# Constant matmuls into a spare PSUM bank, placed where the tensor engine waits in the convolution stage

## What is computed

```python
out = np.einsum('hk,bskhg->bshg', softmax(weight), x_unfolded)   # convolution
logits = x @ w_gate;  e = argmax(logits);  gate_w = softmax(logits)[e]
out = gate_w * (relu(x @ w1[e]) @ w2[e])                         # layer 1
out = gate_w * sigmoid((x @ w_output_gate)[e]) * (relu(x @ w1[e]) @ w2[e])  # layer 2
```

## Time and profile before

| | |
|---|---|
| median of 3 runs | 1430.34 us (1422.12 to 1433.67) |
| the profiled execution | 1426.65 us |
| its span, first to last instruction | 1425.1 us |
| PE busy over the span | 1248.3 us (88%) |
| DVE, ACT, POOL busy | 860.8 (60%), 641.3 (45%), 445.0 us (31%) |
| mean granted TensorE clock | 0.913 |

### The profile page before, as it was taken

One profiled execution on the slowest core, in us unless ns is written; L12 is line 12 of the kernel. 1 busy time (PEld: TensorE's weight loads), 2 busy tenths in 40 slices (PEclk: granted clock), 3 DMA queues, 4 the chain that ended last, 5 costly groups with the idle time before them and its releaser, 6 DMA issues.

```text
span 1425.1 us, 38152 instructions
## 1 busy us (share of the span) xinstructions
PE 1248.3 (88%) x13162; PEld 1169.3 (82%) x13162; DVE 860.8 (60%) x2298; ACT 641.3 (45%) x1126; POOL 445.0 (31%) x476
## 2 busy tenths in 40 slices
PE   2876763299989999999999991999999999999998
PEld 2765663298979998999999990899999999999997
DVE  3787885358978998887777774333333333333332
ACT  3666664045545555554444441333333333333332
POOL 1366777412323333322222222122222222222222
PEclk9666655599999999999999995999999999999999
DMA  8388674928585858561515113462425525125510
GB/s 232 103 254 265 199 224 145 261 65 218 149 235 141 251 146 240 144 203 42 146 40 148 40 35 94 115 156 44 137 63 142 128 64 152 44 44 151 152 44 16
DMA packets 204695, 194.94 MB, mean 137 GB/s; under 512 B 147359, under 2 KB 179771, under 8 KB 199522
## 3 DMA queue, kind: packets, MB, share of 16 engines
q1 hardware_dynamic: 176352, 127.72, 34.8%
q0 software_dynamic: 26096, 64.50, 14.5%
q10 hardware_dynamic: 2194, 2.06, 0.5%
HBM read 101.38 MB, written 70.80 MB: 121 GB/s over the span
## 4 chain that ended last, share of the span: by engine, by line
PE 72%; DVE 12%; DMA 6%; issue 4%; another core or an unknown queue 2%; ACT 2%; POOL 2%; SPq 1%; POOLq 0%; DVEq 0%; ACTq 0%
PE bank L720 70%; DMA wslot<-image 3%; DVE am L943 2%; PE bank L725 2%; POOL rows L466 2%; DVE split L1027 1%; DVE wslot L1054 1%; DVE wam L1012 1%; DVE split L1030 1%; DMA image<-split 1%; DMA stage<-in_moe_w 1%; DVE rowab L952 1%; ACT conv L564 0%; ACT rowt L564 0%
## 5 line engine op out<-in xcount | busy, mean ns | idle before, releaser
L720 PE MATMUL bank<-xT,wslot 128*128 128x256 f16 x5040 | 639.5, 275 | 59.2 <-DMA xT<-rows 50.1
L1114 DVE SCALAR_TENSOR_TENSOR hl<-bank,hh 128x512 f16<-128x512 f32 x504 | 347.7, 690 | 417.6 <-ACT hh L653 372.6
L720 PEld LDWEIGHTS bank<-xT,wslot 128*128 128x128 f16 x5040 | 485.5, 99 | 110.0 <-DMA xT<-rows 50.2
L653 ACT ACTIVATE hh<-bank 128x512 f16<-128x512 f32 x504 | 300.6, 596 | 535.9 <-PE bank L720 529.6
L720 PE MATMUL bank<-wslot,hh 128*128 128x192 f16 x4032 | 541.0, 246 | 0.4 <-DVE hl L1114 0.4
L720 PE MATMUL bank<-wslot,hl 128*128 128x192 f16 x2016 | 496.7, 246 | 0.0
L720 PEld LDWEIGHTS bank<-wslot,hh 128*128 128x128 f16 x4032 | 369.8, 98 | 11.8 <-issue 0.8
L552 POOL DMA_INDIRECT out_tokens<-y,idxt x126 | 122.5, 972 | 416.6 <-ACT y L664 348.6
L487 POOL DMA_INDIRECT rows<-rowt,idxp x126 | 130.1, 1032 | 358.0 <-PE bank L720 197.7
L720 PEld LDWEIGHTS bank<-wslot,hl 128*128 128x128 f16 x2016 | 197.6, 98 | 0.1
L466 POOL DMA_INDIRECT rows<-rowab,idxa x96 | 109.3, 1138 | 61.7 <-issue 46.1
(11 more groups left out here) (137 smaller groups left out, 873.9 us busy)
## 6 DMA issues: line engine op xcount, KB each, us to landing
wslot<-image SPq DMA_DIRECT2D x32, 1024.0 KB
wslot<-image SPq DMA_DIRECT2D x32, 768.0 KB
image<-split POOLq DMA_DIRECT2D x18, 512.0 KB
image<-split SPq DMA_DIRECT2D x8, 1024.0 KB
image<-split POOLq DMA_DIRECT2D x9, 768.0 KB
xw<-in_x SPq DMA_DIRECT2D x4, 1536.0 KB
stage<-in_moe_w SPq DMA_DIRECT2D x8, 768.0 KB
image<-split SPq DMA_DIRECT2D x8, 768.0 KB
```

What stands on the lines that cost most here:

```text
L653: nc.scalar.activation(hh[:, c, :], bank[c][:, :], ACT.Relu).then_inc(hh_out, 1)
L720: return nc.tensor.matmul(o, a, b_, start=start, stop=stop, skip_group_check=True)
L1114: V.scalar_tensor_tensor(hl[:, c, :], bank[c][:, :], 0.0, hh[:, c, :], ALU.max, ALU.subtract).then_inc(hl_out, 1)
```

## The change

A function `fill(count)` is added to PE's program. It runs `count` matmuls with `ident` as the stationary and `tri`, repeated four times, as the moving operand, 128 by 512 float16, into bank 4. Nobody reads bank 4, and the fills neither wait for nor raise a semaphore. They are called at three kinds of places: 12 behind round r = 0 and the ranks, 8 behind round r = 1, and one in each of the eight rounds of transposes and logits, behind the logits. With both, every full step has 28 more matmuls (12 + 8 + 8). The wait for `consts` moves from the first logits to the head of PE's program.

```diff
+FILLS = (12, 8)
...
-        RB, YB = 5, 6
+        FILL, RB, YB = 4, 5, 6
...
+            def fill(count):
+
+                for _ in range(count):
+                    mm(bank[FILL][:, :].rearrange("p (r c) -> p r c", r=4), ident[:, :],
+                       tri[:, :].unsqueeze(1).broadcast_to((P, 4, P)), True, True)
+
+            pe.wait_ge(consts, 2)
             pe.wait_ge(band_loaded, 16)
...
                     if r == 0 and late(n, 2):
                         step_ranks(n - 2)
+                    fill(FILLS[r])
                 if late(n, 1):
                     step_logits(n - 1)
...
                 if not late(n, 1):
                     pe.wait_ge(gate_ready, 1)
-                    pe.wait_ge(consts, 2)
...
                     if r:
                         round_logits(r - 1)
+                    fill(1)
                 round_logits(RTR - 1).then_inc(logit_done, 1)
```

## The result

The changed kernel took 1440.07 us, the median of 20 runs (1431.96 to 1451.42); the kernel before, run beside it, 1432.76 us (20 runs, 1422.0 to 1445.92). The ratio is 1.0069, with a 95% interval of 1.0045 to 1.0092: by the medians 7.3 us slower, by the ratio 10 (6 to 13). The profiled execution took 1440.66 us, its span is 1439.0 us and its mean granted clock 0.940.

The account below looks back on a forecast made before the run. A step was taken as DVE's work plus a 4.2 us wait tied to the scatter, not PE. Terms 0 + 0 + 2.4 + 0.9 = +3.3 us gave 1430.0 or 1433.6, 1432 taken; own range 1424 to 1440, full range 1404 to 1441.

Parts of the forecast that it names:

- Price of a fill: One 128x512 float16 matmul on PE: 0.22 us at full clock, 0.40 us at half.
- The start: First steps, where PE is on the chain: fills delay r = 1 and step 1's transposes; +2.4 us taken.
- 12 fills in a steady step: Behind r = 0 and the ranks: 107.0 to 109.6 us at full clock, hidden before the next round at 112.74; 0.
- The lag does not hang on PE: The 4.2 us between ranks' end and `posm` was read as tied to the running scatter, 25 us behind its start.
- the first rival: The lag hangs on PE and fills remove it: up to 23.3 us faster, 1408 or 1413 us; chance 0.22.
- The idle time before r = 1: Sign that the forecast is right: PE's 5.74 us of idle before that convolution round shrinks to about 3.
- The end. [...] I take 0.9: Last eight rounds of logits: fills delay `idxa` to 245.7 or 247.1, POOL's last scatter starts at 245.64; 0.1 to 1.5 us.
- the upper of the two bounds: Eight fills at the stage's end put logits and ranks 1.8 to 3.2 us later; 3.2 is at half clock.
- One fill per round, eight per step. [...] 0: Steady transposes and logits: at half clock logits end 3.2 us later, DVE 1.0 us late at most, covered by its wait; 0.
- 8 fills behind r = 1: Steady step: fills end at 119.4, transposes 0.7 us late, covered by 0.78 us of slack; 0, at worst 0.7 us.
- From 92.9 to 106.6 us: PE's clock stays at half although PE is busy 13.35 of 13.7 us with transposes and small logits.
- The clock's own gain: Full clock saves up to 2.6 us a round, some 34 us of PE over 13 slow rounds; counted as 0.

Follow-up runs that it names:

- hidden_12: The changed kernel with only the 12 fills behind round r = 0 from step 2 on, against the kernel before: 1414.08 us, ratio 0.9977.
- hidden_12_twice: The 12 fills behind round r = 0 of steps 2 to 7 alone, run once more, against the kernel before: 1416.26 us, ratio 1.0001.
- after_again: The changed kernel, unchanged, run again on a chip with late PE signals, against the kernel before: 1442.2 us, ratio 1.009.
- steady_only: The changed kernel with 168 of 224 fills, only in the steady steps and none at the two ends, against the kernel before: 1418.11 us, ratio 1.0012.
- after_third: The changed kernel with all 224 fills, on a chip without late signals of ranks or logits, against the kernel before: 1419.86 us, ratio 1.0036.
- before_again: The kernel before, unchanged, run again for its trace on a chip with late PE signals: 1434.65 us, ratio 1.0018.
- The separate halves: Against the kernel before: the 168 fills of the steady steps alone, 1418.11 us, 1.0012; the other 56, at the two ends, alone, 1419.13 us, 1.0032.
- load_first: The kernel before with SP issuing the next expert weights' load ahead of the store of the split ones, no fills: 1434.77 us, ratio 1.0021.
- bridge_20: Fills in the steady steps only, with 20 instead of 8 behind round r = 1, against the kernel before: 1416.31 us, ratio 0.9997.
- warm_end_40: 12 fills behind round r = 0 of steps 2 to 7 plus 40 before the last transposes, against the kernel before: 1418.21 us, ratio 0.9998.

## Why the prediction was wrong

The range of 1404 to 1441 us held the 1440.07, by 0.9 us, and the change is within 1% as most of the chance had it. But the forecast was +3.3 us with an own range to 1440, and the measured change is 6 to 13 us. By its steps:

- **Price of a fill: right.** Forecast 0.22 and 0.40 us; measured 0.216 at full clock and, from rounds of 1.48 us with a fill and 1.07 without, 0.41 at half.
- **The start: right.** Forecast +2.4 us and `am` of step 1 at 48.5; it started at 48.49, and the fills there put the first read of ranks 2.35 us later over all traces (1.7 in the profiled pair).
- **12 fills in a steady step: 0, right.** hidden_12 and hidden_12_twice measure 0.9977 and 1.0001. Their level was read wrong: they were to take 2.6 us at full clock, and in after two groups of twelve took 3.68 and 3.93 us. A faster round r = 0 leaves PE standing before the ranks, 2.62 us in that step, and the clock is at half behind it (106.9 to 110.3 us).
- **The lag does not hang on PE: right**, and it bore the forecast: the first rival, with its 0.22, did not happen. In after_again the wait before `posm` occurs six times with 4 us and more, with rounds r = 0 at full clock and fills behind the ranks, and the distance from the scatter's first DMA stays at 25 us through all the experiments. The idle time before r = 1 shrank from 5.74 us to 0.47 rather than 3, partly because the twelve fills took 3.93 us in that step.
- **"The end. [...] I take 0.9": the first step that failed**, a term of the sum mis-sized. It measured 2.5 us over all traces and 4.2 in the profiled pair. Two readings went into it. The clock: PE stands 12 us before the last transposes, and the window from 216 us on in the trace of before would have shown 0.50, so that the upper of the two bounds, 3.2 us, was the one to take. The cover: `idxa` was followed to 247.1 us and set against POOL's start at 245.64, but POOL's first DMA starts 0.9 us behind `idxa` (254.06 to 254.96 in the trace of after), and the trace of before had the same:

```profile
112.27 0.17 DVE L1003 CAST idxa<-pos 112x16 int32<-112x16 f32 x1
113.33 0.96 POOL L466 DMA_INDIRECT rows<-wslot,idxa  x1 [3.95 <-DVE idxa L1003]
```

247.1 + 0.9 - 245.64 is 2.4 us, close to what the end costs. That it is so close is partly luck: the fills made the last logits 2.5 us longer (12.22 against 9.70), not 3.2, and the 0.8 us of cover that POOL's queue gave was there in the trace of before alone; in the other eight traces without fills at the end the last scatter starts 2.1 us behind the eighth read, as soon as `idxa` lets it. The further 1.6 us of the pair are the late signal, which the later logits ran into.

- **"One fill per round, eight per step. [...] 0": failed in one step of six** of the profiled execution, at 3.7 us, and in none of after_again. The sum had DVE "1.0 us late at most", with the wait of 4.2 us behind it. It rested on logits that are read promptly, as they were in the trace of before; that a later logits' signal can fall into the late stretch itself was not asked, although that stretch had been read as tied to the scatter and not to the ranks. The prediction's own 104.0 us for logits at half clock is 18.0 us behind the scatter's first DMA at 86.04, well inside it.
- **8 fills behind r = 1: 0, right in its sum** as far as is known. steady_only, which has them beside others, measures 1.0012, and in the long step the transposes waited for DVE and not for the fills. Its side effect was missed: a faster round before a start that is fixed elsewhere makes the stand longer, and the clock fell behind it.
- **A row was read too simply.** From 92.9 to 106.6 us PE was said to be busy "with transposes and small logits"; from 100.63 on it was the round r = 0. That a light load doesn't bring the clock back rests on the part up to there.
- **The clock's own gain: 0, right.** The Trainium skill ("TensorE: Matmul & The Clock Gate", section "Why this matters for your kernels") advises keeping TensorE busy so that its clock stays up. The clock did go up, from 0.65 to 0.82 in the stage, and the kernel lost: the advice is about PE's speed, and PE's speed isn't what the steady part of the stage waits for. The size of the gain in PE's own time was set too high: 34 us, where 16 rounds of 2.85 us leave 75.4 - 45.6, some 30, to be had, and 23 came.

With 2.4 for the end the sum would have been +4.8 us, which is what the prompt chips show (after_third: 1.0036, 5.1 us). **What stays open** is the rest on the slow-signal chips, where the ratios are 1.0069 and 1.009. In after_again against before_again the stage explains 5.8 us, and no place for more was found, in an execution that was the fastest of its kernel; the expert layers differ between executions by more than the few us in question. The intervals of the two kinds of chip overlap (1.0012 to 1.006 against 1.0045 to 1.0092), so that a larger loss with slow signals is likely, by the long step above, but not shown. The separate halves were measured on prompt chips only.

## What to carry to other kernels

Fill an engine's standing time only where its next start is set elsewhere and late enough, and leave out every place where it is on the chain, above all the first and the last pass of a pipeline: on the chips without late signals 56 of 224 fills made nearly all the loss, by the medians. Before raising an engine's clock, look for the wait that its speed would shorten; here DVE waited for late signals or for a load, and 23 us less of PE bought nothing. Fills that shorten a round also lengthen the stand behind it, and the clock can fall there. When a term is bounded by a clock, read the clock in that very window, and add the hand-over between engines to both sides of a comparison.

## What the runs showed of the hardware

- **PE's signals can arrive 4 to 8 us late, on some chips only.** In before_again the ranks' reader waits 4.2 us in six steps for matmuls that are over; in load_first DVE reads logits 8.5 us after their end (76.37 to 84.86). It occurs in one stretch of each step, whose end lies 25 us behind the first DMA of the running scatter in six traces. On four other chips it never occurred with ranks or logits, and the kernel before is 15 us faster there; how much of that is due to the signals was not separated. What in the chip holds the signal is not known.
- **A clock at half was not brought back by one fill per round, and a full one was kept by it only behind a short stand.** With one fill per round the clock stayed at 0.50 through all rounds in 120.6 to 141.0 and 216.2 to 245.5 us of after. Where the rounds began at 1.00 behind a stand of 2.05 us or less, it stayed there (bridge_20, after_again, six steps of after). Behind 2.50 us and more it fell within the first three rounds, as in after_third behind 3.40 us:

```profile
119.00:122.30 3.30, 1.50 (x20) 1.13 (x21) 3.30 (x4) 1.30 (x3) 2.70 (x2) 1.00 0.18 53
122.40:132.00 9.60, 9.60 (x86) 7.81 (x84) 9.50 (x15) 6.59 (x13) 7.68 (x7) 0.50 0.73 235
```

- **Without fills it fell although PE had hardly stood.** In warm_end_40 PE stood 0.87 us between the 40 fills and the transposes, and the clock fell three rounds later. The Trainium skill ("TensorE: Matmul & The Clock Gate", section "Part 4: PE-mode transpose") says that transposes don't count as PE being busy in the same way; this agrees.
